# Fourier planes laid out by token tile instead of in token order

## The chip, the cores and the metric

The kernel runs on one core of a Trainium2 chip. The metric is the device time of one execution in microseconds; of the kernel before there are three runs, 778.47, 779.72 and 779.95 us, median 779.72. The engines are TensorE (PE; its weight loads are shown apart as PEld), VectorE (DVE), ScalarE (ACT), GpSimd (POOL) and SyncE (SP), which only issues DMAs here.

## What is computed

Attention with hash buckets, then a Fourier mixing block with an MLP, then a gated MLP that mixes tokens. The change lies in the Fourier mixing:

```python
X = np.fft.fft(x, axis=1)          # over 768 tokens
X = np.fft.fft(X, axis=2)          # over 512 features
mixed = np.real(X).astype(np.float32)
u = x + mixed
...                                # layer norm of u, MLP 512 -> 2048 -> 512, residual
```

There are 2 batches, 768 tokens and 512 features, all fp32.

## The kernel before

Matmuls run on pairs of rounded fp32 values: every operand is split into a high part (H, rounded) and a low part (L, the rest), and a product is three matmuls, hi*hi, hi*lo and lo*hi (`mm3`, line 582). The high part comes from a ScalarE copy that rounds, the low part from a VectorE or GpSimd subtraction.

Token numbers are kept in groups of three: token s = 3p + c of a half (384 tokens) lies in partition p of tile c. A batch has T = 6 tiles, TH = 3 per half.

The Fourier mixing has two steps per batch.

**First step** (`first_transform`, over tokens). The input is folded into sums and differences (`fold_tokens`, `fold_features`, `fold_mirrored` on VectorE, one piece on GpSimd), rounded by ScalarE (`fold_hi`: yHL, z0H) and its rest taken by GpSimd (`fold_lo`: yHL, z0L). There are two passes per batch, p = 0 for even and p = 1 for odd token frequencies. Pass n = 2b + p waits for yHL and z0L of its number. A pass makes two groups of two planes each. The four planes are COS0, SIN1, SIN0, COS1; a plane is 128 features by the token frequencies of the pass, at 193 columns (even) or 192 (odd), in a PSUM bank of its group (banks 4 to 7).

**Out of PSUM.** For every group ScalarE copies the two planes to GH, rounded (`transformed_hi`), and VectorE writes the rest to GL (`transformed_lo`). GH and GL have four rows of 386 columns, in the order of the token frequency, so that an even pass writes columns 0, 2, 4 and so on, an odd one 1, 3, 5. When all four groups of a batch are there, `mirrored` (ScalarE, six copies) and `flipped` (VectorE, two) write MH and ML: the same planes backwards, for the frequencies above 384.

**Second step** (`second_transform`, over features). For each token tile j of the batch, 12 pairs of weight load and matmul: the weights are 128 token frequencies of a plane, the streamed operand is the table T2H or T2L with 256 columns. Tile j takes frequencies c, c + 3, c + 6, ... with c = j mod 3 from GH and GL (j < 3) or MH and ML (j >= 3). That is line 822:

```python
rows = slice(c, c + TH * (P - 1) + 1, TH)
```

The result is added to X by VectorE (`residual`), which frees one of four PSUM banks.

TensorE's program goes through the first step of batch 0, its second step, first step of batch 1, the transposes of the normalised tokens for the MLP (`un_transposes(0)`), second step of batch 1, MLP. Engines run their own programs in the order written and meet at semaphores: g_rdy (a group is in PSUM), ghi_done and glo_done (GH, GL written), mir_done and flip_done (MH, ML), s2_rdy (a tile of the second step is done), x_upd (a residual is added), yhi_done and ylo_done (inputs of the first step). On VectorE the folding for batch 1 stands between the work of batch 0's planes: `fold_features(2)`, `flipped(0)`, `fold_mirrored(2)`, `residual(0)`, `fold_features(3)`, `residual(1)`, `fold_mirrored(3)`, then the other residuals.

Of the kernel before, what the change touches and what calls it, by code (L numbers as in the profile page):

```python
# [8 lines left out]
P = 128  # L9
# [6 lines left out]
HALF = S // 2  # L16
T = S // P
TH = T // 2
# [14 lines left out]
KFULL = MROW + 2  # L33
NTC = HALF // 2 + 1
NTP = NTC + 1
QD = DM // 2
GELU_C = float(np.sqrt(2.0 / np.pi))
GELU_K = float(np.sqrt(0.044715))
# [2 lines left out]
F32R = mybir.dt.float32r  # L41
ACT = mybir.ActivationFunctionType
ALU = mybir.AluOpType
AX = mybir.AxisListType

KB = 1024
# [8 lines left out]
def mixer_kernel(nc, q, k, v, proj, w_ch1, w_ch2, w_in, g_ln, w_sg, b_sg, w_out,  # L55
                 t1_hi, t1_lo, t2_hi, t2_lo, out):
    with ExitStack() as ctx:
# [32 lines left out]
        def run(at, *items):  # L90
            placed = []
            for name, shape, dt in items:
                placed.append((name, at, shape, dt))
                at += (4 * int(np.prod(shape[1:])) + 31) // 32 * 32
            return placed

        t1 = run(ZONE, ("T1H", [P, 2, TH, 2, NTP], F32R), ("T1L", [P, 2, TH, 2, NTP], F32R))
        after_t1 = t1[-1][1] + 4 * 2 * TH * 2 * NTP
        t2 = run(196 * KB, ("T2H", [P, 4, QD], F32R), ("T2L", [P, 4, QD], F32R),
                 ("z0H", [P, 2, TH], F32R), ("z0L", [P, 2, TH], F32R), ("flip", [P, 1], F32))  # L100
# [11 lines left out]
        fft = run(after_t1,  # L112
                  ("fold", [P, TH, DM], F32), ("Z", [P, TH, 2, QD], F32), ("Y", [P, TH * 4 * P], F32),
                  ("yHL", [P, 2, 2, TH * 4 * P], F32R)) + run(
                  152 * KB, ("GH", [P, 4, 2 * NTC], F32R), ("GL", [P, 4, 2 * NTC], F32R),
                  ("MH", [P, 4, HALF], F32R), ("ML", [P, 4, HALF], F32R), ("fold2", [P, TH, DM], F32), ("Y2", [P, TH * 4 * P], F32))
        A = layout("a", t1 + attn + t2 + [("W1H", W1H_AT, [P, FT, KT, P], F32R),
                                                    ("W1R", W1L_AT, [P, FT, KT, P], F32)])
        for n, name in enumerate(("qX", "kX", "qP", "kP")):
            A[name] = A["ops"][:, :, n, :]  # L120
        Ff = layout("f", fft)
# [22 lines left out]
        PS = ctx.enter_context(nc.psum_tensor("PS", [P, 8, 512], F32))  # L144


        def sems(text):
            return [sem(n) for n in text.split()]
# [23 lines left out]
        g_rdy, ghi_done, glo_done, mir_done, flip_done, s2_rdy = sems("g_rdy ghi_done glo_done mir_done flip_done s2_rdy")  # L172
# [111 lines left out]
        COS0, SIN1, SIN0, COS1 = range(4)  # L284
# [7 lines left out]
        def tile(j):  # L292
            return slice(j * P, (j + 1) * P)
# [8 lines left out]
        def gated_half(w):  # L302

            return slice((1 - w) * DM, (2 - w) * DM)

        def rd(ap):

            return ap.bitcast(F32)
# [268 lines left out]
        def _(pe):  # L577
            def mm(dst, lhs, rhs, start, stop, **kw):
                return pe.matmul(dst, lhs, rhs, start=start, stop=stop, **kw)  # L579

            def mm3(dst, hi, lo, rhs_hi, rhs_lo, first, last):

                mm(dst, hi, rhs_hi, first, False)
                mm(dst, hi, rhs_lo, False, False)
                return mm(dst, lo, rhs_hi, False, last)
# [195 lines left out]
            def first_transform(b):  # L781

                for p in range(2):
                    n = 2 * b + p
                    pe.wait_ge(yhi_done, 2 * n + 2)
                    pe.wait_ge(ylo_done, 2 * n + 2)
                    for pair in range(2):
                        group = 2 * n + pair
                        if group >= 4:
                            pe.wait_ge(glo_done, group - 3)  # L790
                        for h in range(2):
                            i = 2 * pair + h
                            dst = PS[:, 4 + group % 4, h * NTP:(h + 1) * NTP]
                            sine = int(i in (SIN0, SIN1))
                            for c in range(TH):
                                at = slice((4 * c + i) * P, (4 * c + i + 1) * P)
                                last = mm3(dst, Ff["yHL"][:, p, 0, at], Ff["yHL"][:, p, 1, at],
                                           A["T1H"][:, p, c, sine, :], A["T1L"][:, p, c, sine, :], c == 0, c == TH - 1)
                            if i == SIN0:

                                row = PS[0:1, 4 + group % 4, h * NTP:(h + 1) * NTP]
                                for c in range(TH):
                                    z0H, z0L = A["z0H"][:, p, c:c + 1], A["z0L"][:, p, c:c + 1]
                                    for lhs, rhs in ((z0H, A["T1H"]), (z0H, A["T1L"]), (z0L, A["T1H"])):
                                        last = mm(row, lhs, rhs[:, p, c, 0, :], False, True, skip_group_check=True)
                        last.then_inc(g_rdy, 1)

            def second_transform(b, j):

                a, c = j // TH, j % TH  # L810
                N = T * b + j
                if j == 0:
                    pe.wait_ge(glo_done, 4 * b + 4)
                if j == TH:
                    pe.wait_ge(mir_done, 6 * b + 6)
                    pe.wait_ge(flip_done, 2 * b + 2)
                if b:
                    pe.wait_ge(utl_done, min(j + 1, KT))
                if N >= 4:
                    pe.wait_ge(x_upd, N - 3)  # L820
                hi, lo = (Ff["MH"], Ff["ML"]) if a else (Ff["GH"], Ff["GL"])
                rows = slice(c, c + TH * (P - 1) + 1, TH)
                for r, parts in enumerate(((COS0, SIN0), (COS1, SIN1))):
                    dst = PS[:, N % 4, r * QD:(r + 1) * QD]
                    for n, i in enumerate(parts):
                        last = mm3(dst, hi[:, i, rows], lo[:, i, rows], A["T2H"][:, i, :], A["T2L"][:, i, :], n == 0, n == 1)
                last.then_inc(s2_rdy, 1)
# [156 lines left out]
        def _(act):  # L984
            def copy(dst, src, scale=1.0):
                return act.activation(dst, src, ACT.Copy, scale=scale)  # L986
# [92 lines left out]


            def transformed_hi(b, p, pair):
                group, cnt = 2 * (2 * b + p) + pair, NTC - p
                act.wait_ge(g_rdy, group + 1)
                if b:
                    act.wait_ge(s2_rdy, T)
                copy(Ff["GH"][:, 2 * pair:2 * pair + 2, p:p + 2 * cnt - 1:2],
                     PS[:, 4 + group % 4, 0:2 * NTP].rearrange("m (i t) -> m i t", i=2)[:, :, 0:cnt]).then_inc(ghi_done, 1)

            def mirrored(b):

                act.wait_ge(glo_done, 4 * b + 4)
                if b:
                    act.wait_ge(s2_rdy, T)
                for i in (COS0, SIN1, COS1):
                    for src, dst in ((Ff["GH"], Ff["MH"]), (Ff["GL"], Ff["ML"])):
                        copy(dst[:, i, :], rd(src[:, i, HALF:0:-1]), -1.0 if i == SIN1 else 1.0).then_inc(mir_done, 1)

            for b in range(B):
                for p in range(2):
# [75 lines left out]
        def _(dve):  # L1175
# [136 lines left out]
            def fold_features(n):  # L1312
# [9 lines left out]
                for r, op in enumerate((ALU.add, ALU.subtract)):  # L1322
                    dve.tensor_tensor(Z[:, :, r, :], src[:, :, 0:QD], src[:, :, QD:DM], op).then_inc(fold_step, 1)  # L1323

            def fold_mirrored(n):
# [3 lines left out]

                dve.tensor_tensor(Y[:, :, 0:2, :], Z[:, :, :, 1:P + 1], Z[:, :, :, QD - 1:P - 1:-1], ALU.add).then_inc(fold_step, 1)  # L1330
                dve.tensor_tensor(Y[:, :, 2:4, 1:P], Z[:, :, :, 1:P], Z[:, :, :, QD - 1:P:-1], ALU.subtract).then_inc(fold_step, 1)  # L1331
                dve.memset(Y[:, :, SIN0, 0], 0.0).then_inc(fold_step, 1)
# [3 lines left out]


            def transformed_lo(b, p, pair):
                group, cnt = 2 * (2 * b + p) + pair, NTC - p
                at = slice(p, p + 2 * cnt - 1, 2)  # L1340
                dve.wait_ge(ghi_done, group + 1)
                dve.tensor_tensor(Ff["GL"][:, 2 * pair:2 * pair + 2, at],
                                  PS[:, 4 + group % 4, 0:2 * NTP].rearrange("m (i t) -> m i t", i=2)[:, :, 0:cnt],
                                  rd(Ff["GH"][:, 2 * pair:2 * pair + 2, at]), ALU.subtract).then_inc(glo_done, 1)

            def flipped(b):

                dve.wait_ge(glo_done, 4 * b + 4)
                for src, dst in ((Ff["GH"], Ff["MH"]), (Ff["GL"], Ff["ML"])):
                    dve.tensor_scalar(dst[:, SIN0, :], rd(src[:, SIN0, HALF:0:-1]), A["flip"][:, 0:1], None,  # L1350
                                      ALU.mult).then_inc(flip_done, 1)

            def residual(N):
# [221 lines left out]
```

## Time and profile before

| | |
|---|---|
| median of the runs | 779.72 us |
| span of the profiled execution | 777.5 us |
| TensorE busy, matmuls | 764.8 us, 98% |
| VectorE / ScalarE / GpSimd busy | 403.3 / 276.8 / 201.7 us |
| mean granted TensorE clock | 0.996 of full |
| Fourier steps of both batches | about 286 to 337 us of the span |

The span runs from the first to the last instruction of the profiled execution; the runs' times also hold what lies around it. Time within the span is counted from its start. Matmuls are pipelined, so the time of one pair of load and matmul is read from the distance of starts, not from a duration. PEclk is the TensorE clock that was granted, as a share of 2.4 GHz.

### The profile page before, as it was taken

The numbers are of one execution on the slowest core, as the hardware profiler recorded it, in microseconds if no ns is written. First come the engines' busy times: TensorE is split into PE (matmuls) and PEld (weight loads), VectorE is DVE, ScalarE is ACT, GpSimd is POOL, SyncE is SP. The second block draws the span as 40 slices with busy tenths as digits, with TensorE's granted clock in tenths as the row PEclk, the third lists the DMA queues.
The fourth block names the chain that finished last, engine by engine and source line by source line (L and its number), as shares of the span: only waits on it lengthen the run. The fifth ranks groups of instructions, "written<-read, shape, count | busy, mean of one in ns | idle before, by whom it ended". The sixth has DMA issues, their size and how long they took to land.

```text
span 777.5 us, 12902 instructions
## 1 busy us (share of the span) xinstructions
PE 764.8 (98%) x4614; PEld 704.1 (91%) x4614; DVE 403.3 (52%) x738; ACT 276.8 (36%) x577; POOL 201.7 (26%) x258
## 2 busy tenths in 40 slices
PE   8999999999999999999999999999999999999998
PEld 7889999999999999998999989999999887888886
DVE  7877777777776558531132214112113387337733
ACT  4456666665665533301111111111113453014401
POOL 4133233332243573377000000000013146003300
PEclk9999999999999989999999999999999999999999
DMA  5333323233221500360000000000031000010001
GB/s 116 65 86 87 85 68 84 64 79 88 70 59 29 191 1 1 102 224 1 1 0 0 0 0 1 0 0 0 1 118 59 14 1 0 25 58 0 0 13 67
DMA packets 55569, 36.14 MB, mean 46 GB/s; under 512 B 40048, under 2 KB 48240, under 8 KB 55024
## 3 DMA queue, kind: packets, MB, share of 16 engines
q1 hardware_dynamic: 52720, 26.76, 12.0%
q0 software_dynamic: 2816, 8.94, 4.4%
q8 instruction: 21, 0.34, 0.2%
q14 instruction: 12, 0.10, 0.0%
HBM read 27.03 MB, written 3.15 MB: 39 GB/s over the span
## 4 chain that ended last, share of the span: by engine, by line
PE 90%; DVE 7%; issue 1%; ACT 1%; POOL 1%; DVEq 0%; POOLq 0%; ACTq 0%
PE PS L579 87%; DVE mneg L1227 2%; PE PS L594 1%; DVE ops L1207 1%; DVE Z L1323 1%; PE PS L900 1%; PE PS L846 1%; PE PS L942 1%; PE PS L868 1%; DVE fold L1310 0%; DVE Y L1330 0%; DVE ops L1197 0%; DVE Y L1331 0%; DVE ops L1194 0%; POOL vr L537 0%
## 5 line engine op out<-in xcount | busy, mean ns | idle before, releaser
L579 PEld LDWEIGHTS PS<-vn,E 128*128 128x128 f32 x1152 | 140.9, 192 | 1.6 <-ACT E L1000 1.4
L579 PE MATMUL PS<-vn,E 128*128 128x65 f32 x1152 | 140.6, 271 | 1.2 <-ACT E L1000 1.2
L1413 DVE SCALAR_TENSOR_TENSOR hL<-PS,hH 128x384 fp32r<-128x384 f32 x64 | 35.7, 557 | 201.5 <-ACT hH L1123 201.5
L579 PE MATMUL PS<-ops 98*128 98x384 f32 (+1 forms) x576 | 128.3, 354 | 1.9 <-DVE mneg L1227 1.5
L1227 DVE TENSOR_REDUCE mneg<-PS 128x1 f32<-128x768 f32 x96 | 91.8, 957 | 52.2 <-PE PS L579 51.0
L1123 ACT ACTIVATE hH<-PS 128x384 fp32r<-128x384 f32 x64 | 31.5, 492 | 231.4 <-PE PS L579 231.4
L1000 ACT ACTIVATE E<-PS 128x384 f32<-128x384 f32 x192 | 83.7, 487 | 77.6 <-PE PS L579 76.2
L579 PEld LDWEIGHTS PS<-ops 98*128 98x128 f32 (+1 forms) x576 | 96.5, 190 | 4.0 <-DVE mneg L1227 2.0
L579 PE MATMUL PS<-unTH,W1L 128*128 128x384 f32 x256 | 86.4, 337 | 0.0
L579 PE MATMUL PS<-unTH,W1H 128*128 128x384 f32 x256 | 86.2, 337 | 0.0
L579 PE MATMUL PS<-unTL,W1H 128*128 128x384 f32 x256 | 85.9, 336 | 0.0
L579 PE MATMUL PS<-W2H,hL 128*128 128x512 f32 x192 | 75.9, 395 | 0.0
L579 PE MATMUL PS<-W2L,hH 128*128 128x512 f32 x192 | 75.7, 395 | 0.0
L579 PE MATMUL PS<-W2H,hH 128*128 128x512 f32 x192 | 75.6, 394 | 0.0
L986 ACT ACTIVATE ops<-PS 64x384 fp32r<-64x384 f32 (+1 forms) x96 | 44.8, 481 | 35.9 <-PE PS L579 20.8
L579 PEld LDWEIGHTS PS<-unTH,W1H 128*128 128x128 f32 x256 | 48.1, 188 | 2.6
L579 PEld LDWEIGHTS PS<-unTL,W1H 128*128 128x128 f32 x256 | 48.1, 188 | 2.5
L579 PEld LDWEIGHTS PS<-unTH,W1L 128*128 128x128 f32 x256 | 48.0, 188 | 0.0
L579 PEld LDWEIGHTS PS<-W2H,hL 128*128 128x128 f32 x192 | 36.0, 188 | 7.7
L579 PEld LDWEIGHTS PS<-W2L,hH 128*128 128x128 f32 x192 | 36.0, 188 | 6.0
L579 PEld LDWEIGHTS PS<-W2H,hH 128*128 128x128 f32 x192 | 36.1, 188 | 5.7
L528 POOL TENSOR_TENSOR WinL<-WinR,WinH 128x512 fp32r<-128x512 f32 x8 | 10.3, 1287 | 115.3 <-ACT WinH L986 115.3
(177 smaller groups left out, 1315.1 us busy)
## 6 DMA issues: line engine op xcount, KB each, us to landing
ops<-ops POOLq DMA_DIRECT2D x28, 192.0 KB, 3.0
W1R<-in_moe_w_ch_dram SPq DMA_DIRECT2D x16, 256.0 KB, 2.7
W2R<-in_moe_w_ch_dram SPq DMA_DIRECT2D x4, 1024.0 KB, 6.8
qk<-in_k_dram SPq DMA_DIRECT2D x32, 96.0 KB, 2.7
qk<-in_q_dram SPq DMA_DIRECT2D x32, 96.0 KB, 2.7
vn<-in_v_dram SPq DMA_DIRECT2D x32, 96.0 KB, 2.7
out_dram<-X SPq DMA_DIRECT2D x12, 256.0 KB, 2.1
WsgR<-in_moe_w_sg_dram SPq DMA_DIRECT2D x1, 2304.0 KB, 8.2
```

Source lines behind the costliest of these rows:

```text
L528: pool.tensor_tensor(M2["WinL"][:, c // 2, cols], R1["WinR"][:, c // 2, cols], rd(M2["WinH"][:, c // 2, cols]), ALU.subtract).then_inc(win ...
L579: return pe.matmul(dst, lhs, rhs, start=start, stop=stop, **kw)
L594: last = pe.transpose(PS[:, bank, tile(c)], A["qk"][:, t.slot(3, 2), a * TH + c, :], ident[:, :])
L846: last = pe.transpose(PS[:, un_bank(n, kt), tile(c)], M1["un"][:, c, tile(kt)], ident[:, :])
L868: last = pe.transpose(PS[:, 5 + n % 3, tile(c)], R2["WsgR"][:, r, at:at + TH * (P - 1) + 1:TH], ident[:, :])
L900: last = pe.transpose(PS[:, 6 + j % 2, tile(kt)], M2["xs"][:, j % 2, tile(kt)], ident[:, :])
L942: last = pe.transpose(PS[:, 6 + j % 2, tile(kt)], M2["gated"][:, j % 2, tile(kt)], ident[:, :])
L986: return act.activation(dst, src, ACT.Copy, scale=scale)
L1000: act.activation(A["E"][:, kt % 3, half(a)], PS[:, ST_BANK + a, 0:HALF], ACT.Exp, scale=EXP_SCALE).then_inc(exp_done, 1)
L1123: act.activation(M1["hH"][:, f % 2, :], PS[:, f % 2, 0:HALF], ACT.Relu).then_inc(hhi_done, 1)
L1227: dve.tensor_reduce(A["mneg"][:, s, j:j + 1], PS[:, max_banks(t, j):max_banks(t, j) + 2, 0:HALF], AX.XY, ALU.max, negate=True).then_inc(ma ...
L1413: dve.scalar_tensor_tensor(M1["hL"][:, f % 2, :], PS[:, f % 2, 0:HALF], 0.0, rd(M1["hH"][:, f % 2, :]), ALU.max, ALU.subtract).then_inc(hl ...
```

## The change

GH and GL change their layout. A row now has three regions, one per residue of the token frequency modulo 3, each of 128 columns and a few more (regions begin at columns 0, 261 and 131 for the residues 0, 1 and 2). Within a region the frequencies stand in order, so a token tile of the second step reads 128 neighbouring columns. MH and ML change in the same way: the mirrored planes are three blocks of 128, and tile j takes one block.

For this the copies out of PSUM read every third column of a plane, region by region, and write every second column of a region (the other pass fills the gaps). 192 columns go so, as 3 x 64 per plane. One frequency of each pass doesn't fit this pattern: the last of the even pass (384) and the first of the odd one (1). It is written by an instruction of its own, of two elements per partition (two planes, one column each). Each group now makes two increments of ghi_done and of glo_done, and the thresholds are doubled.

The mirrored copies read the three regions backwards, 128 columns each, and write three blocks.

```diff
+GCOL = P + 3
+GROW = TH * GCOL
+GAT = (0, 2 * GCOL - 1, GCOL)
+GLAST = ((NTC - 1, GAT[0] + P), (0, GAT[1]))
...
+        def frequencies(group):
+
+            p = (group // 2) % 2
+            return transformed(group)[:, :, p:p + HALF // 2].rearrange("m i (w r) -> m i r w", r=TH)
...
+        def spread(planes, group):
+
+            p, pair = (group // 2) % 2, group % 2
+            rows = planes[:, 2 * pair:2 * pair + 2, :].rearrange("m i (r w) -> m i r w", r=TH)
+            return rows[:, :, :, p:p + P - 1:2]
...
+        def mirror_source(planes, i):
+
+            return planes[:, i, 0:TH * (P + 2)].rearrange("m (c w) -> m c w", c=TH)[:, :, P:0:-1]
...
-                rows = slice(c, c + TH * (P - 1) + 1, TH)
+                rows = tile(c) if a else slice(GAT[c], GAT[c] + P)
...
-                copy(Ff["GH"][:, 2 * pair:2 * pair + 2, p:p + 2 * cnt - 1:2],
-                     PS[:, 4 + group % 4, 0:2 * NTP].rearrange("m (i t) -> m i t", i=2)[:, :, 0:cnt]).then_inc(ghi_done, 1)
+                copy(last_spread(Ff["GH"], group), last_frequency(group)).then_inc(ghi_done, 1)
+                copy(spread(Ff["GH"], group), frequencies(group)).then_inc(ghi_done, 1)
...
-                        copy(dst[:, i, :], rd(src[:, i, HALF:0:-1]), -1.0 if i == SIN1 else 1.0).then_inc(mir_done, 1)
+                        copy(by_tile(dst[:, i, :]), rd(mirror_source(src, i)), -1.0 if i == SIN1 else 1.0).then_inc(mir_done, 1)
...
-                dve.wait_ge(ghi_done, group + 1)
-                dve.tensor_tensor(Ff["GL"][:, 2 * pair:2 * pair + 2, at],
-                                  PS[:, 4 + group % 4, 0:2 * NTP].rearrange("m (i t) -> m i t", i=2)[:, :, 0:cnt],
-                                  rd(Ff["GH"][:, 2 * pair:2 * pair + 2, at]), ALU.subtract).then_inc(glo_done, 1)
+                dve.wait_ge(ghi_done, 2 * group + 2)
+                dve.tensor_tensor(spread(Ff["GL"], group), frequencies(group), rd(spread(Ff["GH"], group)),
+                                  ALU.subtract).then_inc(glo_done, 1)
+                dve.tensor_tensor(last_spread(Ff["GL"], group), last_frequency(group), rd(last_spread(Ff["GH"], group)),
+                                  ALU.subtract).then_inc(glo_done, 1)
```

ScalarE, the four groups of batch 0 and the mirrored copies behind them. Before (GH, MH and ML are the planes, PS is PSUM; brackets name the semaphores waited for):

```order
L986 ACTIVATE GH<-PS 128x386 [waits g_rdy] x2
L986 ACTIVATE GH<-PS 128x2x192 [waits g_rdy] x2
L986 ACTIVATE MH<-GH 128x384 [waits glo_done]
L986 ACTIVATE ML<-GL 128x384
L986 ACTIVATE MH<-GH 128x384
L986 ACTIVATE ML<-GL 128x384
L986 ACTIVATE MH<-GH 128x384
L986 ACTIVATE ML<-GL 128x384
```

Now; line numbers have moved by 37:

```order
L1023 ACTIVATE GH<-PS 128x2 [waits g_rdy]
L1023 ACTIVATE GH<-PS 128x6x64
L1023 ACTIVATE GH<-PS 128x2 [waits g_rdy]
L1023 ACTIVATE GH<-PS 128x6x64
L1023 ACTIVATE GH<-PS 128x2 [waits g_rdy]
L1023 ACTIVATE GH<-PS 128x6x64
L1023 ACTIVATE GH<-PS 128x2 [waits g_rdy]
L1023 ACTIVATE GH<-PS 128x6x64
L1023 ACTIVATE MH<-GH 128x384 [waits glo_done]
L1023 ACTIVATE ML<-GL 128x384
L1023 ACTIVATE MH<-GH 128x384
L1023 ACTIVATE ML<-GL 128x384
```

Each group has a copy of two columns ahead of its large one, which is now 6 x 64. The wait for g_rdy moved to the small copy.

VectorE at the same place, with the folding of batch 1 between. Before:

```order
L1342 TENSOR_TENSOR GL<-PS,GH 128x386 [waits ghi_done]
L1310 TENSOR_TENSOR fold<-X 128x1536 [waits fold_step,x_done]
L1342 TENSOR_TENSOR GL<-PS,GH 128x386 [waits ghi_done]
L1323 TENSOR_TENSOR Z<-fold 128x3x256 [waits fold_step,ylo_done,yhi_done]
L1323 TENSOR_TENSOR Z<-fold 128x3x256
L1342 TENSOR_TENSOR GL<-PS,GH 128x2x192 [waits ghi_done] x2
L1350 TENSOR_SCALAR MH<-GH,flip 128x384 [waits glo_done]
```

Now:

```order
L1378 TENSOR_TENSOR GL<-PS,GH 128x6x64 [waits ghi_done]
L1380 TENSOR_TENSOR GL<-PS,GH 128x2
L1347 TENSOR_TENSOR fold<-X 128x1536 [waits fold_step,x_done]
L1378 TENSOR_TENSOR GL<-PS,GH 128x6x64 [waits ghi_done]
L1380 TENSOR_TENSOR GL<-PS,GH 128x2
L1360 TENSOR_TENSOR Z<-fold 128x3x256 [waits fold_step,ylo_done,yhi_done]
L1360 TENSOR_TENSOR Z<-fold 128x3x256
L1378 TENSOR_TENSOR GL<-PS,GH 128x6x64 [waits ghi_done]
L1380 TENSOR_TENSOR GL<-PS,GH 128x2
L1378 TENSOR_TENSOR GL<-PS,GH 128x6x64 [waits ghi_done]
L1380 TENSOR_TENSOR GL<-PS,GH 128x2
L1387 TENSOR_SCALAR MH<-GH,flip 128x384 [waits glo_done]
```

The small subtraction stands behind the large one, ahead of `flipped` (MH, ML). No other instruction has changed its place, on any engine, and TensorE's sequence is the same instruction by instruction.

## Rows read from the trace of the kernel before

**Rows 1.** The page, chain that ended last: share of the span by engine.

```profile
PE 90%; DVE 7%; issue 1%; ACT 1%; POOL 1%; DVEq 0%; POOLq 0%; ACTq 0%
```

**Rows 2.** The chain in order of time, 280 to 345: start, us, what.

```profile
299.37 0.52 ACT GH L986
...
299.92 0.57 DVE GL L1342
...
300.62 22.50 PE PS L579 x162
323.13 1.31 PE PS L846 x12
...
324.85 20.19 PE PS L579 x111
```

**Rows 3.** Timeline of weight loads (PEld): start, us, instruction, count.

```profile
300.59 0.25 PEld L579 LDWEIGHTS PS<-T2H,GH 128*128 128x128 f32 x1 [1.43 <-issue]
...
313.21 0.20 PEld L579 LDWEIGHTS PS<-T1H,yHL 128*128 128x128 f32 x1
...
315.01 0.19 PEld L579 LDWEIGHTS PS<-T1L,yHL 128*128 128x128 f32 x1
...
337.56 0.19 PEld L579 LDWEIGHTS PS<-unTL,W1H 128*128 128x128 f32 x1
...
340.87 0.19 PEld L579 LDWEIGHTS PS<-unTH,W1L 128*128 128x128 f32 x1
...
345.92 0.19 PEld L579 LDWEIGHTS PS<-W2L,hH 128*128 128x128 f32 x1
...
347.77 0.19 PEld L579 LDWEIGHTS PS<-unTH,W1H 128*128 128x128 f32 x1
```

**Rows 4.** Weight loads: group 280 to 345 (mean ns); two lines, ns min/median/max.

```profile
L579 PEld LDWEIGHTS PS<-T2H,GL 128*128 128x128 f32 x24 | 6.3, 264 | 0.0
...
L868 PEld LDWEIGHTS PS<-ident,WsgR x36: 193/201/203, 588.2 to 604.9; 128*128 128x128 f32 x36
...
L846 PEld LDWEIGHTS PS<-ident,un x48: 138/140/143, 322.9 to 540.0; 128*128 128x128 f32 x48
```

**Rows 5.** The mirrored planes' users and makers (by tile); residual additions (groups).

```profile
L579 PEld LDWEIGHTS PS<-T2H,MH x24: 259/260/264, 306.9 to 336.9; 128*128 128x128 f32 x24
...
L986 ACT ACTIVATE MH<-GH x6: 508/537/554, 300.5 to 326.7; 128x384 fp32r<-128x384 f32 x6
...
L1357 DVE TENSOR_TENSOR X<-PS,X 128x512 f32<-128x512 f32 x12 | 8.1, 687 | 8.7 <-PE PS L579 8.7
```

**Rows 6.** Timeline of VectorE, GpSimd, ScalarE, TensorE, 305 to 318, [idle before <-releaser].

```profile
305.96 3.65 DVE L1330 TENSOR_TENSOR Y<-fold 128x768 f32<-128x768 f32 x1
...
308.75 0.91 POOL L489 TENSOR_TENSOR z0L<-Z,z0H 128x3 fp32r<-128x3 f32 x1
...
310.59 1.49 ACT L986 ACTIVATE yHL<-Y 128x1536 fp32r<-128x1536 f32 x1 [5.89 <-DVE Y L1333]
...
315.69 0.20 POOL L489 TENSOR_TENSOR z0L<-fold,z0H 128x3 fp32r<-128x3 f32 x1
...
318.02 0.39 PE L579 MATMUL PS<-T1H,yHL 128*128 128x194 f32 x2
```

**Rows 7.** Small and contiguous instructions: groups, 280 to 345; one row of VectorE's timeline.

```profile
L986 ACT ACTIVATE unTH<-PS 128x384 fp32r<-128x384 f32 x4 | 1.6, 499 | 0.0
...
L986 ACT ACTIVATE z0H<-Z 128x3 fp32r<-128x3 f32 x2 | 0.4, 187 | 0.0
...
316.18 0.32 DVE L1382 BATCH_NORM_AGGREGATE mv<-st 128x2 f32<-128x6 f32 x3
```

**Rows 8.** TensorE before the slow stretch; windows with PEclk, the granted clock.

```profile
284.87 1.60 PE L579 MATMUL PS<-vn,E 128*128 128x65 f32 x12 [1.25 <-ACT E L1000]
...
286.00:293.00 7.00, 7.00 (x37) 6.77 (x37) 3.64 (x7) 0.53 (x1) 6.30 (x5) 0.52 0.00 1
298.00:302.00 4.00, 2.71 (x21) 2.56 (x19) 2.05 (x5) 2.00 (x5) 0.00 (x0) 1.00 0.00 0
```

More of the change, by code:

```diff
@@ L114, in mixer_kernel @@
                   ("yHL", [P, 2, 2, TH * 4 * P], F32R)) + run(
-                  152 * KB, ("GH", [P, 4, 2 * NTC], F32R), ("GL", [P, 4, 2 * NTC], F32R),
+                  152 * KB, ("GH", [P, 4, GROW], F32R), ("GL", [P, 4, GROW], F32R),
                   ("MH", [P, 4, HALF], F32R), ("ML", [P, 4, HALF], F32R), ("fold2", [P, TH, DM], F32), ("Y2", [P, TH * 4 * P], F32))
@@ L304, in gated_half, with transformed, last_frequency, last_spread @@
             return slice((1 - w) * DM, (2 - w) * DM)
+        def transformed(group):
+            return PS[:, 4 + group % 4, 0:2 * NTP].rearrange("m (i t) -> m i t", i=2)
+        def frequencies(group):
+            p = (group // 2) % 2
+            return transformed(group)[:, :, p:p + HALF // 2].rearrange("m i (w r) -> m i r w", r=TH)
+        def last_frequency(group):
+            at = GLAST[(group // 2) % 2][0]
+            return transformed(group)[:, :, at:at + 1]
+        def spread(planes, group):
+            p, pair = (group // 2) % 2, group % 2
+            rows = planes[:, 2 * pair:2 * pair + 2, :].rearrange("m i (r w) -> m i r w", r=TH)
+            return rows[:, :, :, p:p + P - 1:2]
+        def last_spread(planes, group):
+            pair, at = group % 2, GLAST[(group // 2) % 2][1]
+            return planes[:, 2 * pair:2 * pair + 2, at:at + 1]
+        def mirror_source(planes, i):
+            return planes[:, i, 0:TH * (P + 2)].rearrange("m (c w) -> m c w", c=TH)[:, :, P:0:-1]
+        def by_tile(plane):
+            return plane.rearrange("m (c w) -> m c w", c=TH)
         def rd(ap):
@@ L789, in first_transform @@
                         if group >= 4:
-                            pe.wait_ge(glo_done, group - 3)
+                            pe.wait_ge(glo_done, 2 * (group - 3))
                         for h in range(2):
@@ L812, in second_transform @@
                 if j == 0:
-                    pe.wait_ge(glo_done, 4 * b + 4)
+                    pe.wait_ge(glo_done, 8 * b + 8)
                 if j == TH:
@@ L1081, in transformed_hi @@
             def transformed_hi(b, p, pair):
-                group, cnt = 2 * (2 * b + p) + pair, NTC - p
+                group = 2 * (2 * b + p) + pair
                 act.wait_ge(g_rdy, group + 1)
@@ L1085, in transformed_hi @@
                     act.wait_ge(s2_rdy, T)
-                copy(Ff["GH"][:, 2 * pair:2 * pair + 2, p:p + 2 * cnt - 1:2],
-                     PS[:, 4 + group % 4, 0:2 * NTP].rearrange("m (i t) -> m i t", i=2)[:, :, 0:cnt]).then_inc(ghi_done, 1)
+                copy(last_spread(Ff["GH"], group), last_frequency(group)).then_inc(ghi_done, 1)
+                copy(spread(Ff["GH"], group), frequencies(group)).then_inc(ghi_done, 1)
             def mirrored(b):
-                act.wait_ge(glo_done, 4 * b + 4)
+                act.wait_ge(glo_done, 8 * b + 8)
                 if b:
@@ L1338, in transformed_lo @@
             def transformed_lo(b, p, pair):
-                group, cnt = 2 * (2 * b + p) + pair, NTC - p
-                at = slice(p, p + 2 * cnt - 1, 2)
-                dve.wait_ge(ghi_done, group + 1)
-                dve.tensor_tensor(Ff["GL"][:, 2 * pair:2 * pair + 2, at],
-                                  PS[:, 4 + group % 4, 0:2 * NTP].rearrange("m (i t) -> m i t", i=2)[:, :, 0:cnt],
-                                  rd(Ff["GH"][:, 2 * pair:2 * pair + 2, at]), ALU.subtract).then_inc(glo_done, 1)
+                group = 2 * (2 * b + p) + pair
+                dve.wait_ge(ghi_done, 2 * group + 2)
[3 more added lines that the diff above has]
+                                  ALU.subtract).then_inc(glo_done, 1)
             def flipped(b):
-                dve.wait_ge(glo_done, 4 * b + 4)
+                dve.wait_ge(glo_done, 8 * b + 8)
                 for src, dst in ((Ff["GH"], Ff["MH"]), (Ff["GL"], Ff["ML"])):
-                    dve.tensor_scalar(dst[:, SIN0, :], rd(src[:, SIN0, HALF:0:-1]), A["flip"][:, 0:1], None,
+                    dve.tensor_scalar(by_tile(dst[:, SIN0, :]), rd(mirror_source(src, SIN0)), A["flip"][:, 0:1], None,
                                       ALU.mult).then_inc(flip_done, 1)
```

## The prediction

> **What bounds the kernel now.** I read the shares of the chain that ended last first [rows 1]: TensorE's own work is 90% of the span, so what counts is whether a stage gives TensorE less to do or lets it start sooner. Then I read the same chain, in order of time, over the Fourier steps of both batches [rows 2]. TensorE stops in it at the border from the first step to the second: ScalarE copies the last planes out of PSUM (299.37, 0.52 us), VectorE subtracts (299.92, 0.57), and the second step begins at 300.62 in batch 0. In batch 1 twelve transposes stand there as well (323.13), and it begins at 324.85. Between these places the chain is TensorE alone.
>
> Third, the starts of the weight loads in order of time [rows 3]. The second step of batch 0 has 6 tiles x 4 planes x 3 products = 72 pairs of load and matmul and lasts from 300.59 to 313.21: 12.62/72 = 0.175 us a pair, for 256 columns streamed. Contiguous weights take, at the same full clock:
>
> - 194 columns: 313.21 to 315.01, 16 pairs, 0.1125 us
> - 384 columns: 337.56 to 340.87, 19 pairs, 0.174 us
> - 512 columns: 345.92 to 347.77, 8 pairs, 0.231 us
>
> So 256 columns cost here what 384 cost elsewhere. What sets this step apart is its weights, read at every third element (line 822): a load takes 264 ns [rows 4], against 190 ns for the contiguous ones in rows 3. Transposes show the same far from here: 201 ns for weights at a step of three (L868), 140 ns for contiguous ones (L846) [rows 4].
>
> **What a pair costs after the change.** Every load of the second step will read 128 neighbours. The line through 384 and 512 columns gives 0.174 - (0.231 - 0.174) = 0.117 us at 256. Columns at 2.4 GHz plus what the two rows take above that (0.174 - 0.160 = 0.014, 0.231 - 0.213 = 0.018) give 0.121 to 0.125. I take 0.120. Bounds: 0.1125, where the row at 194 columns shows the load of 128 columns to be the limit, and 0.175, no change, if the step is not the cause. The saving is 0.055 x 72 = 4.0 us of TensorE work per batch; 4.5 by the lower bound.
>
> The Trainium skill (Advanced Engine Details and Errata, section Memory Cachelines) says that SBUF has 16-byte lines and that a line wants at least two hits; fp32 elements 12 bytes apart mostly have one. By that rule the trace agrees, 264 against 190 ns. The same section gives PSUM lines of two fp32 values and wants neighbours there, which speaks against this change, since the step of three moves into a read of PSUM; its price is the second rival below.
>
> **Batch 1 keeps all 4.0 us.** Behind its second step the first MLP block follows at once (337.56 is its second load, and nothing but TensorE is in the chain). Two covers shrink, and both hold [rows 5]. Tile 3 needs the mirrored planes: their first load is 306.9 - 300.6 = 6.3 us after the step's start, and will be 36 x 0.12 = 4.3 us after it; ScalarE's six copies begin at 300.5 and take at most 6 x 0.554 = 3.3 us. Each tile's residual addition takes 0.69 us on VectorE, a tile 12 x 0.12 = 1.44 us.
>
> **Batch 0 loses half of it again.** Behind it comes the first step of batch 1, whose inputs come from VectorE, ScalarE and GpSimd in turn [rows 6]. Its first pass needs GpSimd's z0L, done at 308.75 + 0.91 = 309.66. The second pass needs the next z0L, done at 315.69 + 0.20 = 315.89: VectorE builds Y from 305.96, ScalarE rounds it at 310.59 after waiting 5.89 us for it, and GpSimd subtracts. TensorE is not in this chain: the two residuals that VectorE does on the way have long been released. TensorE comes to the passes at 313.21 and 318.04 now (a pass is 36 pairs and 9 one-row products, 4.83 us; the second begins with the second half of the pair at 318.02). After the change the second step would start 0.2 late (next paragraph), at 300.82, and end at 300.82 + 8.64 = 309.46. The first pass waits until 309.66 + 0.2 + 0.05 = 309.9 and ends at 314.7. The second waits for 315.89 + 0.2 + 0.05 = 316.14. The 0.05 is my allowance for a semaphore; rows 2 have 0.03 between ScalarE's end (299.89) and VectorE's start. Gain in batch 0: 318.04 - 316.14 = 1.9 us in place of 4.0, with two new stalls of TensorE, 0.4 and 1.4 us.
>
> **What is added.** Eight times a ScalarE copy and a VectorE subtraction of two elements per partition. In six cases TensorE is still at work in the first step beside them, and nothing waits. Those of each batch's last group stand in the chain. ScalarE's small copy goes ahead of the large one. Alone it would take 0.187 us like z0H; ScalarE's instructions overlap by some 0.1 (0.52 us long, and six of them in 3.3 or less), so I count 0.1. VectorE's comes behind its large one: three small ones need 0.32 us, 0.08 to 0.1 each [rows 7]. Together 0.2 us per batch; bounds 0 (both hidden in the large ones) and 0.187 + 0.16 = 0.35. In batch 0 this 0.2 also pushes the mirrored planes and the chain of GpSimd, as counted above.
>
> The large copies read PSUM at a step of three and write SBUF at a step of two. They wrote so before, too, and took 0.52 us against 0.499 for the contiguous unTH [rows 2, 7]: a step on the SBUF side is nearly free for ScalarE. No row shows a long read of PSUM at a step. Bounds: nothing, or the share that the step adds to a weight load, 74/190 = 39% of 0.52 + 0.57, 0.43 us per batch. I take nothing, since the nearest row is a ScalarE copy with a step. The mirrored copies read three runs of 128 backwards in place of one of 384; the elements are as many, and the cover is 1 us.
>
> **Sum.** Batch 0: 1.9. From there to the second step of batch 1 only the second 0.2 comes in: 1.7. Then 4.0: in all 5.7 us. The profiled span of 777.5 becomes 771.8. The median of the runs, 779.72, lies 2.2 above that span, start and end of the execution around it, which the change leaves alone: 779.72 - 5.7 = 774.0 us. The terms' own bounds: 0.5 less by 0.1125, and 2 x (0.15 + 0.43) = 1.2 more by dearer copies, 773.5 to 775.2; with half the runs' spread (778.47 to 779.95), 772.8 to 775.9.
>
> **Rivals.**
>
> *The clock falls at a new stall.* TensorE waited 1.25 us before 284.87, with runs of 65-column matmuls on both sides, and from 286 to 293 it was granted 0.52 of full speed, mostly 1.2 GHz [rows 8]. The new 1.4 us stall at 314.7 could do the same. Against it: the stall before 300.62 is as long and stands between denser matmuls, and the clock stayed at 1.00. Price: in these 7 us ran 37 matmuls, which at the full clock take 4.83 x 37/45 = 4.0, so 3.0 us are lost: 777.0.
>
> *Reading PSUM at a step is dear.* The large copies double: 1.09 us more per batch at the border, in batch 0 through GpSimd's chain. 5.7 - 2.2 = 3.5: 776.2.
>
> *The step moves from where it is free to where it costs (slower).* If 0.175 us belongs to this matmul and not to its load, nothing is gained, and the doubled copies and the small ones put 1.3 us into each border: 779.72 + 2.6 = 782.3. It is slower by over 0.2% once the two borders together grow by 1.6 us. Against it stand 0.1125 and 0.174 on either side of 256 columns. With cheap copies the same case gives 779.72 + 0.4 = 780.1, within 0.2%.
>
> *Batch 0 keeps its gain too.* If the chain of VectorE and GpSimd moves up with TensorE, 2.1 us more: 771.9. Against it: VectorE is at Y from 305.96 on, when TensorE is still at tile 2 or 3, and ScalarE waits for VectorE alone.
>
> **Chances.** As summed 0.70; clock 0.08; doubled copies 0.09; no gain in the loads 0.08 (0.04 slower, 0.04 within 0.2%); full gain in batch 0 0.05. The range for 8 in 10 is 772.6 to 777.0: it takes in the forecast with its bounds and the two mild rivals, and leaves out the last two cases. 0.2%, 1.6 us, is about the least that a measurement of this kernel can tell from no change. Faster by more than that: 0.70 + 0.08 + 0.09 + 0.05 = 0.92, less 0.02 for several losses at once, 0.90; within 0.06; slower 0.04.
>
> **What would show it.** Right: loads of the second step near 190 ns; pairs 0.12 us apart, 8.6 us for the 72 of a batch; TensorE idle until GpSimd's z0L twice, 0.4 us before the first pass of batch 1 and 1.4 before its second; large copies near 0.52 and 0.57 us; clock 1.00 throughout 310 to 340; the second step of batch 1 beginning at 323.1. Wrong: loads still near 264 ns, large copies over 0.75 us, a clock under 1.00 after the stalls, or no stall for z0L.

## The result

The changed kernel takes 772.12 us (median of 6 runs, 771.26 to 773.60) against 779.09 (6 runs, 776.98 to 779.95): 0.9916 of the time, 95% interval 0.9902 to 0.9930. It is faster, as forecast, but 772.12 lies 0.5 below the range of 772.6 to 777.0.

The span of the profiled execution went from 777.5 to 771.8 us, by the 5.7 that the terms summed to. That this says less than it seems to is the main lesson below. The chain over the Fourier steps after the change, start, us, what [rows 2]:

```profile
299.40 0.59 ACT GH L1023 x2
299.99 0.02 issue
300.01 0.56 DVE GL L1378
300.57 0.08 DVE GL L1380
300.65 0.14 issue
300.78 8.61 PE PS L616 x72
309.39 0.89 issue
310.29 5.05 PE PS L616 x45
315.33 1.19 issue
316.52 5.05 PE PS L616 x45
321.57 1.31 PE PS L883 x12
322.88 0.55 issue
323.43 21.61 PE PS L616 x140
```

Both second steps are shorter: 8.61 us in batch 0, and in batch 1 from 323.43 on. The two long gaps marked "issue", 0.89 and 1.19 us, are the new stalls of TensorE ahead of the two passes of the next first step; the forecast had 0.4 and 1.4. The second step of batch 1 begins at 323.43, where 323.1 had been expected. The weight loads of the second step, groups by shape [rows 4], and their starts [rows 3]:

```profile
L616 PEld LDWEIGHTS PS<-T2H,GL 128*128 128x128 f32 x24 | 4.5, 188 | 0.0
...
L616 PEld LDWEIGHTS PS<-T2H,ML 128*128 128x128 f32 x24 | 4.5, 188 | 0.0
```

```profile
300.86 0.19 PEld L616 LDWEIGHTS PS<-T2L,GH 128*128 128x128 f32 x1
...
304.90 0.19 PEld L616 LDWEIGHTS PS<-T2H,GL 128*128 128x128 f32 x1
...
305.02 0.19 PEld L616 LDWEIGHTS PS<-T2H,MH 128*128 128x128 f32 x1
...
309.01 0.19 PEld L616 LDWEIGHTS PS<-T2H,ML 128*128 128x128 f32 x1
```

A load takes 188 ns instead of 264, as contiguous loads do elsewhere. The pairs from GH and GL are (304.90 - 300.86)/34 = 0.119 us apart, those from MH and ML (309.01 - 305.02)/35 = 0.114; for both kinds 0.120 had been taken. The copies out of PSUM and what was added, VectorE and ScalarE groups [rows 5, 7]:

```profile
L1378 DVE TENSOR_TENSOR GL<-PS,GH 128x384 fp32r<-128x384 f32 x8 | 4.4, 551 | 7.3 <-ACT GH L1023 7.3
...
L1387 DVE TENSOR_SCALAR MH<-GH,flip 128x384 fp32r<-128x384 f32 x2 | 1.2, 606 | 0.0
...
L1380 DVE TENSOR_TENSOR GL<-PS,GH 128x2 fp32r<-128x2 f32 x8 | 1.2, 150 | 0.0
```

```profile
L1023 ACT ACTIVATE GH<-PS 128x384 fp32r<-128x384 f32 x8 | 4.2, 525 | 0.0
...
L1023 ACT ACTIVATE GH<-PS 128x2 fp32r<-128x2 f32 x8 | 1.4, 171 | 20.0 <-PE PS L616 20.0
```

The read of PSUM at a step of three costs nothing here: 525 ns for ScalarE (526 before the change) and 551 for VectorE (554 before). The small instructions cost a little less than estimated (in the chain, 0.59 us for both ScalarE copies in place of 0.52, and 0.08 for VectorE's). The surprise is `flipped`: 606 ns instead of 414, for a read of three runs backwards. ScalarE's mirrored copies make the same change of pattern and hardly differ (542 ns for MH, 532 before); why VectorE's do is open. `flipped` delays the fold for batch 1, and by that GpSimd's z0L [rows 6]:

```profile
309.27 0.91 POOL L526 TENSOR_TENSOR z0L<-Z,z0H 128x3 fp32r<-128x3 f32 x1
...
316.22 0.20 POOL L526 TENSOR_TENSOR z0L<-fold,z0H 128x3 fp32r<-128x3 f32 x1
```

z0L now ends at 310.18 and 316.42, 0.52 and 0.53 us later than before, where 0.2 had been summed.

### The profile page after: what moved, and what is told of

It is laid out like the page before. It is cut to its first block, busy times and chain, and to the rows that moved or that the text cites. A ratio compares the mean times of both kernels' runs of the same rounds, so it can differ in the third digit from the quotient of the medians.

```text
span 771.8 us, 12918 instructions
## 1 busy us (share of the span) xinstructions
PE 756.7 (98%) x4614; PEld 695.7 (90%) x4614; DVE 404.3 (52%) x746; ACT 277.4 (36%) x585; POOL 201.9 (26%) x258
## 4 chain that ended last, share of the span: by engine, by line
PE 90%; DVE 7%; issue 1%; ACT 1%; POOL 1%; DVEq 0%; POOLq 0%; ACTq 0%
PE PS L616 86%; DVE mneg L1264 2%; PE PS L631 1%; DVE ops L1244 1%; DVE Z L1360 1%; PE PS L937 1%; PE PS L979 1%; PE PS L883 1%; PE PS L905 1%; DVE fold L1347 0%; DVE Y L1367 0%; DVE ops L1234 0%; DVE Y L1368 0%; DVE ops L1231 0%; POOL vr L574 0%
```

## The experiments

Each time is a median; the runs of the kernel before on the same chip have a median of 778.5 to 779.4. Since the question was where the level of 772.12 came from, the first four runs look at the runs' own spread.

**The clock of the single runs.** The two kernels once more, unchanged.

> The changed kernel once more, for the spread of its runs and the granted clock of each. Theory A: the trace was summed rightly (5.7 us), and the measured level lies lower because the profiled runs of both kernels contained the 7 us at half clock near 286 us, which most other runs have for a shorter time. Then time falls with mean clock over the runs: about 771.3 at 1.000, 772.1 at 0.998, 773.6 at 0.995, and the difference to the kernel before is 5.7 us between runs of one clock. Rival B: the change gives more than the trace sum, 6.5 to 7 us, at equal clocks too.

> The kernel before once more, for the same purpose. Theory A: its runs spread from 777 (clock 1.000) over 778 (0.998) to 779.5 (0.995), and more of them are at 0.995 than of the changed kernel. Rival B: 779 at clocks like those of the changed kernel. Against itself the ratio is 1.000.

Measured: the changed kernel 773.29 us (6 runs), the kernel before 779.37 (23 runs) in one series and 778.96 (12 runs) in another. Ordered by each run's mean granted clock (its time minus its span is 1.8 or 1.9 us in every run):

| mean clock | before, us (runs) | changed, us (runs) |
|---|---|---|
| 1.000 | 776.94 to 777.05 (3) | 771.24 to 771.26 (2) |
| 0.998 | 777.3 (2) | 772.0 to 772.2 (4) |
| 0.995 to 0.996 | 778.4 to 778.6 and 779.3 to 779.4 | 773.2 to 773.6 (6) |
| 0.992 to 0.993 | 779.5 to 780.0 | none |

At the full clock the difference is 777.01 - 771.25 = 5.8 us. That is theory A, and B falls: the work itself shrank by what the trace sum said. The other rows can't be paired like this, since one mean clock stands for falls in different places: at 0.998 the two kernels are 5.2 us apart. What moves the medians is how often, and how long, the clock is down. The first six runs of the changed kernel had mostly 0.998, the six of e1 mostly 0.996; that alone is the step from 772.12 to 773.29. Windows of the kernel before, in the profiled execution of the forecast and in that of e2 (the clock is the third number from the end):

```profile
286.00:290.00 4.00, 4.00 (x22) 4.00 (x21) 1.60 (x5) 0.00 (x0) 3.38 (x4) 0.53 0.00 0
...
290.00:298.00 8.00, 8.00 (x64) 7.67 (x64) 7.04 (x6) 1.59 (x3) 3.64 (x2) 0.81 0.01 3
...
298.00:302.00 4.00, 2.71 (x21) 2.56 (x19) 2.05 (x5) 2.00 (x5) 0.00 (x0) 1.00 0.00 0
```

```profile
286.00:290.00 4.00, 4.00 (x25) 4.00 (x24) 1.66 (x5) 0.00 (x0) 3.38 (x4) 0.60 0.00 0
...
298.00:302.00 4.00, 2.80 (x14) 2.83 (x15) 3.46 (x9) 3.37 (x8) 0.00 (x0) 0.81 0.00 0
...
302.00:306.00 4.00, 4.00 (x23) 4.00 (x22) 4.00 (x5) 1.28 (x2) 2.64 (x1) 0.77 0.00 0
```

In the first the clock is down from 286 to about 293 only. In the second it is down for a shorter time, from 287 to about 290, and a second time from about 300.5 to 303.9, in the second Fourier step. The profile that the forecast rested on did not show this second fall. The lowest level, 0.993, would fit runs with the long first fall and the second one; no such run was profiled, so this is not shown. No run of the changed kernel went below 0.995.

**Filling the waits.** Idle matmuls into a PSUM bank that nobody uses at that time, ahead of the last head's last values.

```diff
                     if kt == 0 and t.has(-1):
+                        if not t.looped and t.it == LOOPS and t.u == SLOTS:
+                            pe.wait_ge(tab1_in, 32)
+                            for _ in range(7):
+                                mm(PS[:, 7, 0:2 * NTP], ident_r[:, :],
+                                   A["T1H"][:, 0, 0, :, :].rearrange("p s n -> p (s n)"), True, True)
                         values(t, -1, T - 1)
```

> The kernel before with 7 idle matmuls of 388 columns into an unused bank, in the wait of 1.25 us ahead of the last head's last values (near 283.6 us). Nothing of the computation is left out. Theory A: TensorE stays at full clock from 286 to 293, all runs are at 0.999 to 1.000 clock, the time is 776.8 with a spread under 0.7 us. Rival B (the level has another cause than the clock): no change of spread or time, 779. If the fill itself delays the values: up to 0.3 us on top.

> The changed kernel with the same 7 matmuls. Theory A: 771.2, clock 0.999 to 1.000, and 5.7 us below the kernel before with fill. Rival B: 772, and 6.5 to 7 us below it.

Measured: 777.42 (777.09 to 777.57, 12 runs) and 771.15 (771.09 to 771.29, 4 runs). The spread of 3 us is gone from the kernel before, of 2 us from the changed one. So the fall at 286 belongs to the wait of 1.25 us [rows 8] and costs 2.1 to 2.4 us where it is long (773.3 and 773.6 less 771.2). But e3 still has 0.997 or 0.998 in all its runs, where 0.999 to 1.000 and 776.8 had been expected, and the difference is 6.3, not 5.7. The windows of e3, then of e4:

```profile
286.00:290.00 4.00, 4.00 (x40) 3.95 (x39) 2.28 (x7) 0.53 (x1) 3.30 (x4) 1.00 0.01 2
...
298.00:302.00 4.00, 4.00 (x20) 4.00 (x21) 3.64 (x8) 3.90 (x8) 0.01 (x1) 0.57 0.00 0
```

```profile
286.00:290.00 4.00, 4.00 (x40) 3.95 (x39) 2.31 (x7) 0.59 (x2) 3.38 (x4) 1.00 0.00 0
...
298.00:302.00 4.00, 3.72 (x31) 3.75 (x32) 3.96 (x10) 3.45 (x7) 0.00 (x0) 1.00 0.00 0
```

With the loads at a step of three the clock falls behind the stall between the steps (0.57 from 298 to 302); with contiguous loads it stays at 1.00. The first matmul of the second step in e3 and in e4, with TensorE's idle time before it in brackets:

```profile
297.83 0.42 PE L579 MATMUL PS<-T2H,GH 128*128 128x256 f32 x1 [2.01 <-DVE GL L1347]
...
298.28 0.36 PE L616 MATMUL PS<-T2H,GH 128*128 128x256 f32 x1 [2.15 <-DVE GL L1385]
```

This stall is 2.0 us in e3 and 2.15 in e4, against 1.3 and 1.4 in the profiled executions of the two kernels with the long fall at 286: the first step ends earlier at the full clock, but VectorE's planes don't come as much earlier. So the stall hides some 0.7 us of a long fall, which costs 2.4 us where the forecast's rival had priced one at 3.0. This second stall filled too, in the kernel before:

```diff
                 if j == 0:
+                    if b == 0:
+                        for _ in range(7):
+                            mm(PS[:, 1, 0:2 * NTP], ident_r[:, :], ...)
                     pe.wait_ge(glo_done, 4 * b + 4)
```

> The kernel before with the fill of e3 and 7 such matmuls more in the wait of 1.3 us between the first and the second step of batch 0. Nothing is left out. In e3 the clock fell to half from about 298.8 to 302 in every run (0.998). Theory A: the loads at a step of three keep TensorE so thin behind this stall that the clock falls, which the changed kernel avoids; with the stall filled it stays at 1.000 and the time is 776.95, 0.45 below e3, 5.8 above e4. Rival B: the clock falls anyway, or the time stays at 777.4.

Measured: 776.70 (776.45 to 776.79, 6 runs), clock 0.999 to 1.000:

```profile
298.00:302.00 4.00, 4.00 (x24) 4.00 (x24) 4.00 (x9) 3.91 (x8) 0.01 (x1) 1.00 0.00 0
```

Theory A holds, with 0.7 us below e3 where 0.45 was expected, and 5.55 above e4 where 5.8 was. The second fall is a cost that goes with the old layout; e3's runs all have a mean clock that fits it, and e5 below, with the old layout in GH and GL, has it in its profile (0.67 from 298 to 302). A fall is rarer with the new layout, not excluded: two of four runs of e6, two of four of e7 and one of four of e10 are at 0.998 and 0.5 to 0.9 us slower than their fellows. None of those was profiled, so where the clock fell in them is not known.

**Where batch 0's share goes.** Both kernels have the first fill; e5 has the old layout in GH and GL, e6 the new one but the old step for MH and ML.

```diff
 e5, on the kernel before
-                rows = slice(c, c + TH * (P - 1) + 1, TH)
+                rows = tile(c) if a else slice(c, c + TH * (P - 1) + 1, TH)
...
+            return planes[:, i, HALF:0:-1].rearrange("m (w c) -> m c w", c=TH)
 e6, on the changed kernel
-                rows = tile(c) if a else slice(GAT[c], GAT[c] + P)
+                rows = slice(c, c + TH * (P - 1) + 1, TH) if a else slice(GAT[c], GAT[c] + P)
```

> Half of the change, with the fill of e3: GH and GL keep the token order, only MH and ML are written tile by tile (ScalarE's and VectorE's mirrored copies read at a step of minus three), so 36 of the 72 loads per batch are contiguous; no small copies, no PSUM read at a step. Theory A (batch 0 is cut off by GpSimd's z0L, batch 1 is not): 36 x 0.061 = 2.2 us in batch 1, 1.6 in batch 0, in all 3.8 below e3: 773.6. Rival B (gain in proportion to the loads): half of the 6.3 between e3 and e4, 774.3. If the copies at a step are dear, they show over 0.6 us each and MH is waited for.

> The changed kernel with the fill (e4), but the 36 loads per batch from MH and ML are read at a step of three again; the second half of each batch's second step then multiplies wrong rows, all else is computed. Theory A: batch 0 has 2.2 us more of TensorE work and shows none of it, because TensorE then reaches the second pass of the next first step just as z0L comes (316.3 for 316.5); batch 1 pays 2.2: 771.15 + 2.2 = 773.4, and the two stalls of batch 0 are gone from the trace. Rival B: 4.4 us slower, 775.5.

Measured: e5 773.29 (773.10 to 773.31, 4 runs), 0.3 us below theory A; e6 773.72 (4 runs), its two runs at full clock 773.29 and 773.33, the other two 774.11 and 774.18. Of e4 and then of e6, the chain in order of time:

```profile
298.28 8.61 PE PS L616 x72
...
306.89 0.90 issue
...
307.79 5.03 PE PS L616 x45
...
312.82 1.20 issue
...
314.02 5.05 PE PS L616 x45
...
320.93 24.11 PE PS L616 x152
```

```profile
298.29 15.58 PE PS L616 x117
...
314.01 5.04 PE PS L616 x45
...
320.91 24.26 PE PS L616 x142
```

e6 has 2.2 us more work in batch 0's second step, no stall behind it, and begins the second pass at 314.01 as e4 does at 314.02. Its 2.15 us come from batch 1 alone. So half of the loads could stay at a step of three in batch 0 without any cost: the gain there was cut off by the chain over VectorE, ScalarE and GpSimd, as forecast. e5 reaches, with half of the loads, 4.1 of the 6.3 us; of the 6.3, 0.7 is the second fall, which e5's clock still makes. Rival B's 774.3 is out. It also shows what a step of three costs ScalarE on reading SBUF:

```profile
L999 ACT ACTIVATE MH<-GH x6: 732/760/770, 298.0 to 323.7; 128x384 fp32r<-128x384 f32 x6
```

760 ns against 537 [rows 5].

**The chain over GpSimd taken away.** `fold_lo(2)` and `fold_lo(3)` move from GpSimd to VectorE, behind residual(1) and residual(3); the first fill is in.

```diff
             residual(1)
+            fold_lo(2)
             fold_mirrored(3)
-            for j in range(2, T):
+            residual(2)
+            residual(3)
+            fold_lo(3)
+            for j in range(4, T):
                 residual(j)
```

> The changed kernel with the fill, and the subtractions for yHL and z0L of batch 1 done by VectorE in place of GpSimd. Nothing is left out. Theory A (the chain over GpSimd ate batch 0's gain): VectorE's Y for the last pass is no longer slowed by GpSimd (0.95 instead of 3.66 us), z0L is ready by 308.5 and 313.6, TensorE has no stall there, second pass from 314.3 instead of 316.5: 2.2 us less than e4, 769.0. Rival B: VectorE becomes late with the residuals, or something else holds batch 1 back, 770.5 or more.

Measured: 769.64 (769.30 to 769.94, 4 runs), 769.3 and 769.4 at full clock: 1.8 us less than e4, of 2.2 expected. TensorE has no stall ahead of the two passes any more. The chain gets shorter on VectorE too. Its fold for the second pass [rows 6], which ran beside GpSimd's subtraction, takes 0.95 us with GpSimd idle:

```profile
305.86 0.95 DVE L1370 TENSOR_TENSOR Y<-fold 128x768 f32<-128x768 f32 x1
```

It took 3.65 us before, and 3.67 in e4. So 2.7 us of the chain were this slowdown, which the forecast had taken as it stood. The missing part of the 2.2, in the chain of e7:

```profile
315.05 0.90 POOL rstd L541
...
315.98 1.47 DVE un L1441 x3
...
317.49 1.53 PE PS L886 x12
...
319.25 25.80 PE PS L614 x161
```

TensorE waits for the normalised tokens (VectorE's un, behind GpSimd's rstd) before its transposes, since the first step now ends too early for them.

**A version faster than both.** The statistics for these tokens are taken ahead of residuals 4 and 5, and the regions of GH and GL are 132 columns wide.

```diff
-GCOL = P + 3
+GCOL = P + 4
...
             fold_lo(3)
+            dve.wait_ge(x_upd, TH)
+            statistics(0)
+            dve.wait_ge(ln_st, TH)
+            aggregate()
             for j in range(4, T):
                 residual(j)
```

> e7 with two edits; nothing is left out. VectorE takes the layer norm's statistics of the first three tiles right behind z0L, ahead of the residuals 4 and 5, since in e7 TensorE waited 0.83 us for the normalised tokens, behind GpSimd's rstd. And the regions of GH and GL are one column wider (132), so two of three begin at a multiple of 16 bytes. Theory A: the wait goes, 0.8 us; pairs of tiles 0 and 2 at 0.114 us like those of MH, tile 1 at 0.119 (24 pairs x 0.005 x 2 = 0.2 us): 768.3 at full clock. Rival B: the 0.005 has another cause (ScalarE and VectorE busy beside it), all GH pairs stay at 0.119; or the statistics push residuals that something waits for: 769.3.

Measured: 769.21 (769.15 to 770.06, 4 runs), 0.9878 of the kernel before (0.9861 to 0.9894): rival B's 769.3, not theory A's 768.3. Its chain:

```profile
315.61 1.38 DVE un L1445 x3
...
317.03 1.53 PE PS L886 x12
...
318.80 26.24 PE PS L614 x162
```

The second step of batch 1 begins 0.45 us earlier than in e7, less than the 0.8 hoped for, since the normalised tokens are still late by a little. And theory A on alignment is wrong: in e10 the pairs of all six tiles are 0.118 to 0.119 us apart, those of MH too, which were at 0.114 in e7 with the same alignment to 16 bytes. That takes 0.17 us back per batch. The other engines' work does not explain it: in batch 0's second step all engines do the same in e7 and e10. What differs there is where things lie in SBUF, but not by the rule that was tried; the cause is open.

**The load by itself.** Steps of two and four in the kernel before.

```diff
+                rows = slice(c, c + 2 * (P - 1) + 1, 2)
...
+                        at = (i % 2) * HALF + c
+                        four = slice(at, at + 4 * (P - 1) + 1, 4)
+                        wH, wL = [x[:, four] for x in flat] if a else (hi[:, i, rows], lo[:, i, rows])
```

> The kernel before, with the loads of the second step read at a step of two from GH and GL and at a step of four from MH and ML (both take wrong columns, so the second step multiplies wrong rows; all else is computed). It measures the load alone. Theory A (16-byte lines, two hits wanted, a load pays for each line beyond 64): step two costs 188 ns and pairs 0.12 us; step three has 96 lines and 262 ns, so step four has 128 lines: 188 + 2 x 74 = 336 ns, pairs near 0.24 us. Rival B (any step over one costs the same): 262 ns at both. Rival C (a step over two costs once): 188 and 262 ns.

Measured, one execution, loads at a step of four, then two:

```profile
L579 PEld LDWEIGHTS PS<-T2H,ML 128*128 128x128 f32 x24 | 8.0, 333 | 0.0
...
L579 PEld LDWEIGHTS PS<-T2H,GL 128*128 128x128 f32 x24 | 4.7, 198 | 0.0
```

With the loads of the two kernels that makes 188, 198, 262 and 333 ns for steps of one to four, and pairs at 0.120 us (step two) and 0.235 (step four). The numbers are near theory A's 188 and 336; B and C fall. That a load pays by the line is a model that fits these four numbers, no more; the 10 ns that a step of two does cost are not in it.

## Why the prediction came out as it did

- *The step slows the load, the load paces the pair.* Right: 264 to 188 ns, and e8 adds steps of two and four. By what the Trainium skill says of SBUF lines (Advanced Engine Details and Errata, section Memory Cachelines: at least two hits on a line of 16 bytes), fp32 loads at a step of two should be free and at a step of three not. The trace agrees nearly: 198 ns (e8) and 262 (kernel before) against 188.
- *A pair costs 0.120 us.* A little too dear: 8.36 us for 72 pairs (323.40 to 331.76), 0.116. In batch 1 the 72 pairs took 12.62 us before as well (324.82 to 337.44), so it gained 12.62 - 8.36 = 4.26, not 4.0.
- *Batch 0 keeps 1.9 us.* The mechanism was right (e6, e7), the size was not: 318.04 - 316.52 = 1.5. Of the missed 0.4, z0L's extra lateness is 0.33, and it comes from `flipped` (2 x 0.19 us), whose backward read of three runs had been set at nothing.
- *Added instructions, 0.2 us per border.* Nearly right: TensorE's pause at the border grew by 0.13 us in batch 0 (1.29 to 1.42) and by 0.14 in batch 1 (0.41 to 0.55). The stall of PSUM reads at a step did not come (525 and 551 ns): the warning for PSUM in that section of the Trainium skill, made for matmuls, is not borne out for these copies.
- *The sum, 5.7.* 1.42 + 4.26 = 5.7 in the profiled executions; the two errors of size, 0.3 too much in batch 0 and 0.3 too little in batch 1, cancelled, which is luck. Between runs at full clock it is 5.8.
- *The level, 774.0.* This step failed. The sum was laid on the median of three runs, 779.72, taken as 2.2 us "around the span" of 777.5 "which the change leaves alone". The surroundings are 1.8 us in every run, so a run like the profiled one takes 779.35, and less 5.7 that is 773.65; the changed kernel's profiled execution measured 773.60 (span 771.8). The other 0.4 were another state of the clock; runs near 779.7 have a mean clock of 0.992 or 0.993, the profiled execution 0.996. So 0.4 of the 1.9 us between 774.0 and 772.12 is the base; the other 1.5 is the clock.
- *The clock, a rival only.* It had been treated as something that could only fall anew in the changed kernel (the rival at 777.0). In truth it falls in most runs of both kernels at 286, for a longer or shorter time: five of the six runs behind 772.12 were at 0.998 or 1.000, the profiled one at 0.995. With that wait filled the changed kernel takes 771.15 (e4). In the kernel before the clock falls a second time near 300, in runs that the one profile did not show. The change takes away that second fall, 0.7 us where it was filled (e3 to e9), so up to that much of the difference of the medians, 7.0. Whether the median lay inside the range was then luck: 772.12 is 0.5 below it, by the mix of clock states that six runs happened to have, and six others gave 773.29, inside it.
- *The rivals.* Clock falling at the new stalls: no, 1.00 from 310 to 340 in the profiled execution. Dear PSUM: no. Step moved to where it costs: no. Batch 0's full gain: no, and e7 shows what it takes.

## What to carry to other kernels

Read a TensorE stage by the distance of its starts; where it exceeds what the columns ask for, look at the step of the weights, and move a step of three or more into the copy out of PSUM, where it cost nothing here. Before a gain is credited, follow the producers of the next stage: what they don't give up, the stage won't. Look there for an instruction that takes several times what the same one takes elsewhere in the trace: here that was VectorE's fold beside GpSimd, 3.65 us for 0.95. And before a forecast is laid on a median of runs, know the clock states of those runs: here they spread one kernel by 3 us, half of the effect.

## What the runs showed that was not expected

- VectorE's fold of 128x768 fp32 from SBUF: 3.65 us beside GpSimd's subtraction, 0.95 with GpSimd idle (e7). The residual additions, which read PSUM, take 0.69 us either way (313.54 and 303.01 in the kernel before).
- Loads of 128 fp32 columns: 188, 198, 262, 333 ns at steps of one to four.
- ScalarE reading SBUF at a step of minus three: 760 ns for 384 columns, against 537 in one run backwards; reading PSUM at a step of three: 525, no more than contiguous with the same write. VectorE's tensor_scalar: 414 ns for one run backwards, 606 for three runs, 740 at a step of minus three.
- A wait of 1.3 to 2.1 us of TensorE can halve its clock or not, and more than its length decides. Behind the stall of 1.3 us between the steps, with pairs at 0.175 us after it, the clock stayed up in one profiled execution of the kernel before and fell in the other (e2). Behind 2.0 us and such pairs (e3) it fell in the profile, and all 12 runs have a mean clock of 0.997 or 0.998. Behind 2.15 us and pairs at 0.12 (e4) it stayed up in the profile; one of the four runs is at 0.998, and no slower. Seven idle matmuls of 388 columns in the wait at 284 kept the clock at 1.00 from 286 on, and are worth 2 us here.
